# A convolution and two MLPs on one core: TensorE's program without a loop, and a reordered start

## The reference

```python
x (2, 4096, 192), weight (8, 7); moe_w_in (192, 2048), moe_w_out (2048, 192), and a second pair moe2_*
w = softmax(weight)                                   # one row of 7 taps for each group of 24 columns
x = sum over k of w[head, k] * x_padded[:, s + k]     # 6 rows of zeros ahead of each sequence
h = x @ w_in ;  g = maximum(0.01 * h, h) ;  x = g @ w_out
h = x @ w_in2 ; g = where(h >= 1, h, where(h <= -1, 0, (h + 1) ** 2 / 4)) ; out = g @ w_out2
```

## Time and profile before

| | us |
|---|---|
| median of 3 runs | 1184.76 (1181.87 to 1184.83) |
| the profiled execution | 1185.6 |
| its span, first to last instruction | 1183.9 |
| PE busy | 1161.6 (98%) |
| DVE busy | 896.6 (76%) |
| ACT busy | 798.2 (67%) |
| POOL busy | 50.6 (4%) |

### The profile page before, as it was taken

The page is one execution under the profiler, slowest core; times in us unless marked ns, Lnnn a source line. Parts: engine busy times, 40 slices in busy tenths (PEclk is TensorE's granted clock), DMA queues, the critical chain, the costliest instruction groups (busy, mean ns, idle before and its releaser), DMA issues.

```text
span 1183.9 us, 26785 instructions
## 1 busy us (share of the span) xinstructions
PE 1161.6 (98%) x9764; PEld 1142.1 (96%) x9764; DVE 896.6 (76%) x1509; ACT 798.2 (67%) x1473; POOL 50.6 (4%) x76
## 2 busy tenths in 40 slices
PE   9999999999999999999999999999999999999998
PEld 7879999999999999999999999999999999999997
DVE  6788777678777887768877678777777867878665
ACT  6768667485675857748577575765757657586685
POOL 5650000000000000000000000000000000000000
PEclk9999999999999999999999999999999999999999
DMA  5430100101001010010100101001010100100001
GB/s 136 109 61 2 18 11 1 30 2 25 4 2 30 2 28 2 2 29 2 28 2 10 22 2 28 1 12 19 1 28 1 25 7 1 28 1 16 1 1 28
DMA packets 114484, 22.43 MB, mean 19 GB/s; under 512 B 106128, under 2 KB 114320, under 8 KB 114320
## 3 DMA queue, kind: packets, MB, share of 16 engines
q1 hardware_dynamic: 114000, 20.07, 9.4%
q10 hardware_dynamic: 320, 0.26, 0.1%
HBM read 14.02 MB, written 6.29 MB: 17 GB/s over the span
## 4 chain that ended last, share of the span: by engine, by line
PE 93%; DVE 2%; ACT 2%; SPq 1%; issue 1%; POOL 0%; DMA 0%; POOLq 0%; ACTq 0%
PE hidden L385 7%; PE acc_main L477 5%; PE acc_main L479 5%; PE acc_main L475 5%; PE acc_edge L469 5%; PE acc_edge L467 5%; PE hidden L397 5%; PE hidden L401 5%; PE hidden L399 5%; PE hidden L404 5%; PE hidden L377 5%; PE hidden L381 5%; PE hidden L379 5%; PE acc_edge L441 5%; PE acc_edge L438 5%; PE acc_main L447 5%
## 5 line engine op out<-in xcount | busy, mean ns | idle before, releaser
L638 ACT CAST g_hi<-g 128x512 fp32r<-128x512 f32 x512 | 299.6, 618 | 311.5 <-PE acc_main L479 271.1
L848 DVE TENSOR_TENSOR g_lo<-g,g_hi 128x512 fp32r<-128x512 f32 x512 | 336.1, 690 | 143.9 <-ACT g_hi L638 138.9
L385 PE MATMUL hidden<-op_edge,w_edge 64*128 64x512 f32 x768 | 262.3, 395 | 0.0
L842 DVE SCALAR_TENSOR_TENSOR g<-hidden,pre 128x512 f32<-128x512 f32 x256 | 176.7, 690 | 105.7 <-ACT pre L626 102.8
L377 PE MATMUL hidden<-op_hi,w_main 64*128 64x512 f32 x512 | 202.3, 395 | 14.4 <-DVE g L837 13.8
L381 PE MATMUL hidden<-op_hi,w_main 64*128 64x512 f32 x512 | 202.0, 394 | 0.0
L441 PE MATMUL acc_edge<-g_lo,w_out 64*128 64x512 f32 x508 | 200.7, 395 | 1.0 <-DVE g_lo L848 0.8
L379 PE MATMUL hidden<-op_lo,w_main 64*128 64x512 f32 x512 | 201.7, 394 | 0.0
L397 PE MATMUL hidden<-op_hi,w_main 64*128 64x512 f32 x512 | 201.3, 393 | 0.0
L401 PE MATMUL hidden<-op_hi,w_main 64*128 64x512 f32 x512 | 201.3, 393 | 0.0
L399 PE MATMUL hidden<-op_lo,w_main 64*128 64x512 f32 x512 | 200.8, 392 | 0.0
(11 more groups left out here) (111 smaller groups left out, 2786.0 us busy)
## 6 DMA issues: line engine op xcount, KB each, us to landing
x_in<-in_x_dram SPq DMA_DIRECT2D x68, 64.0 KB, 2.2
out_dram<-y_main SPq DMA_DIRECT2D x64, 64.0 KB, 1.9
stage<-in_moe_w_out_dram SPq DMA_DIRECT2D x16, 192.0 KB, 3.5
x_in_edge<-in_x_dram SPq DMA_DIRECT2D x68, 32.0 KB, 1.9
out_dram<-y_edge SPq DMA_DIRECT2D x32, 64.0 KB, 1.8
stage<-in_moe_w_in_dram SPq DMA_DIRECT2D x15, 128.0 KB, 2.3
stage<-in_moe_w_in_dram SPq DMA_DIRECT2D x30, 64.0 KB, 3.0
stage<-in_moe_w_in_dram ACTq DMA_DIRECT2D x1, 128.0 KB, 3.2
```

Of the source, the lines that this page charges most:

```text
L385: done = nc.tensor.matmul(h[:], w_edge[l][top, i - 3, cols], op_edge[l][b][top, :], start=False, stop=False)
L638: nc.scalar.copy(g_hi[c % SLOTS][:], g[c % SLOTS][:]).then_inc(g_hi_ready, 1)
L848: nc.vector.tensor_tensor(g_lo[c % SLOTS][:], g[c % SLOTS][:], g_hi[c % SLOTS][:].bitcast(F32), ALU.subtract).then_inc(g_lo_ready, 1)
```

## The change

The diff has these parts.

- PE's program has no loop: the 7 passes are written out. The other engines keep theirs.
- The first warm-up has 12 matmuls instead of 8, the second 2 instead of 3, and the third (8, ahead of job 0) is gone.
- In `opening`, chunk 0 begins with its two edge passes and the edge pass of chunk 1, then come the passes with `op_hi`, and the ones with `op_lo` last. Each waits for its own operand. DVE instead of ACT makes two of the three edge operands of tile 0, in `edge_lo`, with a new semaphore `edge_tops_ready`.
- The two tap matmuls write to two banks, and ACT copies them one by one.
- Loads: the fourth quarter of the first `x_main` and `w_out` of piece 0 go from SP's queue to ACT's; the rest of piece 0 is issued behind the exponential; SP loads piece 2 ahead of the main part of tile 1.
- Jobs 0 and 1: the work for tile 1 and for the second MLP of tile 0 is laid at other chunks (`main_hi` at 5, `edge_hi` at 9, `edge_top` at 11, main taps at 0 to 3, edge taps at 2 to 8, `main_lo` at 7; in job 1 `take_edge` and what follows four chunks earlier, main taps from 9 instead of 7). Three main taps instead of two, and no edge taps, stand ahead of job 0. In the loop's jobs `turn`, `at` and `taps_at` give the chunks of before (`between_sum` at 10, and so on).

```diff
 AHEAD = 3
-WARM = 8
-WARM_ON = (3, 8)
+WARM = 12
+WARM_ON = 2
 EARLY = (0, 1)
...
         def _(sp):
-            def load_x_main(b, pos):
+            def load_x_main(b, pos, parts=P // Q):
                 group = b * (S // Q) + pos * GROUPS
-                for q in range(P // Q):
+                for q in range(parts):
                     sp.dma_start(x_in[b][Q * q:Q * (q + 1), :].rearrange("r (g c) -> r g c", c=Q),
...
-            load_x(EVEN, 0)
-            s, _, _, rows, _ = piece_parts(0)
-            sp.dma_start(rows, w_out_dram[0][:, 0:PC, :]).then_inc(stage_loaded[0], 16)
+            load_x_main(EVEN, 0, parts=P // Q - 1)
+            load_x_edge(EVEN, 0)
             load_weights(1)
+            load_weights(2)
             load_x_main(ODD, 0)
-            load_weights(2)
             load_x_edge(ODD, 0)
...
-            def top_first(job, c, i):
+            def top_first(job, c, i, first=0):
                 n, l, t, b = job["n"], job["layer"], job["t"], job["b"]
                 k = CHUNKS * n + c
                 cols = slice(c * P, (c + 1) * P)
                 h = hidden[c % SLOTS]
+                last = 1 if first else 4 - c % 2
+                done = None
+                if i == first and is_number(n, 0) and c % PC == 0:
+                    pe.wait_ge(weights_ready, c // PC + 1)
+                if first and c == 0:
+                    if i == first:
+                        pe.wait_ge(edge_tops_ready, 1)
+                    if i == 0:
+                        pe.wait_ge(main_rounded, 1)
+                    if i == 1:
+                        pe.wait_ge(first_main_ready, 1)
                 if i == 0:
-                    if is_number(n, 0):
-                        if c == 0:
-                            pe.wait_ge(first_main_ready, 1)
-                        if c % PC == 0:
-                            pe.wait_ge(weights_ready, c // PC + 1)
-                    elif c == 0:
+                    if c == 0 and not is_number(n, 0):
                         pe.wait_ge((op1_ready, op2_ready)[l], t + 1)
                     if reached(k, SLOTS):
                         pe.wait_ge(g_ready, k - SLOTS + 1)
-                    nc.tensor.matmul(h[:], w_main[l][top, 0, cols], op_hi[l][b][top, :], start=True, stop=False)
+                    nc.tensor.matmul(h[:], w_main[l][top, 0, cols], op_hi[l][b][top, :], start=first == 0, stop=False)
                 elif i == 1:
-                    nc.tensor.matmul(h[:], w_main[l][top, 0, cols], op_lo[l][b][top, :], start=False, stop=False)
+                    done = nc.tensor.matmul(h[:], w_main[l][top, 0, cols], op_lo[l][b][top, :], start=False, stop=False)
                 elif i == 2:
                     nc.tensor.matmul(h[:], w_main[l][top, 1, cols], op_hi[l][b][top, :], start=False, stop=False)
                 else:
-                    if is_number(n, 0) and c == 0 and i == 3:
-                        pe.wait_ge(op1_ready, 1)
                     done = nc.tensor.matmul(h[:], w_edge[l][top, i - 3, cols], op_edge[l][b][top, :],
-                                            start=False, stop=False)
-                    if i == 4 - c % 2:
-                        done.then_inc(hidden_top_made, 1)
+                                            start=i == first, stop=False)
+                if i == last:
+                    done.then_inc(hidden_top_made, 1)
...
                     last = c % 2 == 0
+                    if is_number(n, 0) and c == 0:
+                        pe.wait_ge(op1_ready, 1)
                     done = nc.tensor.matmul(h[:], w_edge[l][bottom, 0, cols], op_edge[l][b][bottom, :],
...
-                for i in range(5):
-                    top_first(job, 0, i)
+                for c, i in (0, 3), (0, 4), (1, 3), (0, 0), (0, 2), (1, 0), (0, 1):
+                    top_first(job, c, i, first=3)
                 for i in range(2):
-                    top_first(job, 1, i)
-                for i in range(2):
-                    top_first(job, 1, i + 2)
+                    top_first(job, 1, 2 - i, first=3)
                     bottom_first(job, 0, i)
...
             for a in (0, 1):
-                last = nc.tensor.matmul(acc_main[0][:, a * TAPS:(a + 1) * TAPS], head_of[:, a, :], taps_head[:],
-                                        start=True, stop=True)
-            last.then_inc(taps_spread, 1)
-
-            keep_warm(WARM_ON[0])
+                nc.tensor.matmul((acc_main, acc_edge)[a][0][:, 0:TAPS], head_of[:, a, :], taps_head[:],
+                                 start=True, stop=True).then_inc(taps_spread, 1)
+
+            keep_warm(WARM_ON)
             pe.wait_ge(x_turned, 1)
             for i in range(TAPS):
                 pe.wait_ge(diag_ready, i + 1)
                 last = nc.tensor.matmul(hidden[3][:], diag[i], x_main[0][:, i:i + T], start=i == 0, stop=i == TAPS - 1)
             last.then_inc(main_convolved, 1)
-            keep_warm(WARM_ON[1])
-            all_jobs(pe, run)
+            for job in first_jobs:
+                run(job)
+            for j in range(PASSES):
+                for job in loop_jobs(j):
+                    run(job)
+            for job in last_jobs:
+                run(job)
             for i in range(10):
...
                 act.wait_ge(edge_tapped, TAPS * (t + 1))
-                nc.scalar.copy(e[0:EDGE, 0:HALF], conv[0:EDGE, :]).then_inc(edge_hi_ready, 1)
+                if t > 0:
+                    nc.scalar.copy(e[0:EDGE, 0:HALF], conv[0:EDGE, :]).then_inc(edge_hi_ready, 1)
                 nc.scalar.copy(top[EDGE:P, HALF:T], conv[EDGE:P, :]).then_inc(edge_hi_ready, 1)
-                nc.scalar.copy(e[0:EDGE, HALF:T], conv[EDGE:P, :]).then_inc(edge_hi_ready, 1)
+                if t > 0:
+                    nc.scalar.copy(e[0:EDGE, HALF:T], conv[EDGE:P, :]).then_inc(edge_hi_ready, 1)
...
                         round_weights(AHEAD + PIECES - 1 + c // PC)
+                    if is_number(n, 0) and c == 1:
+                        move_half(job["load"])
+                    if is_number(n, 0) and c == 5:
+                        main_hi(job["finish"])
                     if is_number(n, 0) and c == 9:
-                        main_hi(job["finish"])
                         edge_hi(job["finish"])
+                    if is_number(n, 0) and c == 11:
                         edge_top(job["finish"])
-                    if job["prev"] and job["prev"][0] == LEAKY and c == 9:
+                    turn = 5 if is_number(n, 1) else 9
+                    if job["prev"] and job["prev"][0] == LEAKY and c == turn:
                         take_edge(n - 1, 1 - job["a"])
                         round_between(job["prev"], n - 1, 1 - job["a"])
-                    if job["prev"] and job["prev"][0] == LEAKY and c == 11:
+                    if job["prev"] and job["prev"][0] == LEAKY and c == turn + 2:
                         top_smooth(job["prev"])
...
                         move_halo(job["load"])
-                    if job["load"] and c == job["at"] + 2 and not is_number(n, 0):
+                    if job["load"] and c == 6 and not is_number(n, 0):
                         move_half(job["load"])
             act.dma_start(taps_raw[:], weight).then_inc(taps_loaded, 16)
-            s = piece_parts(0)[0]
-            act.dma_start(s[:, 0:PW], w_in_dram[0][0:P, 0:PW]).then_inc(stage_loaded[0], 16)
+            act.dma_start(x_in[EVEN][P - Q:, :].rearrange("r (g c) -> r g c", c=Q),
+                          x_rows[:, 0:GROUPS, P - Q:P]).then_inc(x_loaded[EVEN], 16)
             act.wait_ge(taps_step, 2)
             nc.scalar.activation(taps_exp[:], taps_sub[:], ACT.Exp).then_inc(taps_exp_ready, 1)
+            s, _, _, rows, _ = piece_parts(0)
+            act.dma_start(s[:, 0:PW], w_in_dram[0][0:P, 0:PW]).then_inc(stage_loaded[0], 16)
             for r in (0, EDGE):
                 act.dma_start(s[r:r + EDGE, PW:2 * PW], w_in_dram[0][P:D, 0:PW]).then_inc(stage_loaded[0], 16)
             act.wait_ge(taps_spread, 1)
-            nc.scalar.copy(taps[:], acc_main[0][:, 0:2 * TAPS].rearrange("p (a k) -> p a k", a=2)).then_inc(taps_ready, 1)
+            nc.scalar.copy(taps[:, 0, :], acc_main[0][:, 0:TAPS]).then_inc(taps_ready, 1)
             act.wait_ge(same_step, 3)
             act.wait_ge(taps_ready, 1)
             for i in range(TAPS):
                 nc.scalar.activation(diag[i], same, ACT.Copy, scale=taps[:, 0, i:i + 1]).then_inc(diag_ready, 1)
-                if i == 3:
+                if i == 0:
+                    act.wait_ge(taps_spread, 2)
+                    nc.scalar.copy(taps[:, 1, :], acc_edge[0][:, 0:TAPS]).then_inc(taps_ready, 1)
+                    act.dma_start(rows, w_out_dram[0][:, 0:PC, :]).then_inc(stage_loaded[0], 16)
+                if i == 2:
                     move_half((0, EVEN, 0))
             round_weights(0)
+            round_weights(1)
             edge_hi((0, EVEN, 0))
             main_hi((0, EVEN, 0))
             edge_top((0, EVEN, 0))
```

(52 more changed lines are left out.)

## The result

| | before | after |
|---|---|---|
| median, us | 1183.85 (4 runs) | 1162.58 (4 runs, 1162.14 to 1162.92) |
| the profiled execution | 1185.6 | 1162.36 |
| its span | 1183.9 | 1160.6 |
| PE busy | 1161.6 (98%) | 1151.9 (99%) |
| job 2 starts | 85.50 | 83.50 |

The ratio is 0.9816 (95% interval 0.9803 to 0.9829): 21.3 us less by the medians. The forecast was 1159.5, the range 1156 to 1167. Of the 23.3 us by which the span is shorter, 21.1 lie between the start of job 2 and the job behind the loop (993.17 instead of 1014.24 us), 2.0 in the start, 0.2 behind the loop.

The account below looks back on a forecast made before the run. TensorE (PE) was taken as the bound, busy 1161.6 of 1183.9 us. From 1185.6 us, 21.2 for the loop and 4.1 for the start gave 1160.3, less 0.8 for the median: 1159.5, range 1156 to 1167.

Parts of the forecast that it names:

- The loop: PE's 7 passes: PE waits for its own code after six jumps back; writing them out takes off 21.2 us.
- the surplus: Loop time above full rate, 21.2 us: six jumps at about 2.5 us and four slow-clock stretches at about 1.5 us.
- another 0.8 us: Taken off the sum of 1160.3 because the median of three lay 0.8 us below the profiled execution.
- The straight code is fetched in time: PE's written-out passes: code 7 times as long is fetched at the loop body's rate, at no cost.
- The rival in which it isn't: PE's straight code not fetched in time: 1328 us if each of about 80 blocks showed 2.1 us; chance 0.03.
- The cover of ACT's and DVE's jumps: Pass starts: DVE's first `g` stays 1.1 us ahead of PE's chunk 4; cost zero, without cover up to 8 us.
- The warm-up: Start: warm-up 8 to 12 lies on the path, costs 1.25 us; split tap banks return 0.25, convolution ends 1.0 later.
- larger start: Rival: convolution 1.0 to 1.3 us earlier, all waits of jobs 0 and 1 gone; start 6.5, time 1157; chance 0.12.
- DVE in front of the first `g`: Start of job 0: DVE's 3.0 us list after `op_lo` gives first `g` at 18.2 to 18.85; chunk 4 0.7 us earlier.
- The spreading: Jobs 0 and 1, chunk 4 to job 2: moving work to other chunks wins 3.4 of 3.8 us lost.
- My sum for ACT: Jobs 0 and 1: pre, cast and weights at 1.1 us each plus 1.3 us on top stay near 4.4 per pair.
- The start in all: Everything before job 2: 0.7 plus 3.4 gives 4.1 us won, between 2 and 6.5.

Follow-up runs that it names:

- the two pairs of kernels: Kernel before against itself with only PE's 7 passes written out (1163.91 us); changed kernel against itself with PE's loop put back (1181.37 us).
- the short loops that need no fetching: Changed kernel plus six 4-turn PE loops of 16 to 1400 matmuls behind its last product; three idles each with 1000 and 1400, none in the four shorter.

## Why the prediction was right or wrong, point by point

**The loop: right, in mechanism and size.** The sum gave 21.2 us for the passes, the two traces 21.1 (1014.24 to 993.17). The wait's name was VectorE, its cause PE's code: shown by the kernel before with only PE straight, and by the short loops that need no fetching. By the medians of the two pairs of kernels the loop is worth 18.8 and 20.9 us. One thing was overlooked: how many jumps are followed by a slow stretch changes from run to run (four in the profile of before, three with the loop put back). I had subtracted the surplus of an execution with four of them, at 1.5 us each, and then another 0.8 us because it lay that much above the median. But these stretches go with the jumps: the four runs before spread over 3.0 us, the four after over 0.8, and there the median lies 0.2 us above the profiled execution. That is 1.0 of the 3.1 us between the forecast and the measured median.

**The straight code is fetched in time: right** (4 packets, no gap). The rival in which it isn't fell by 4 packets in 65 us and no idle time behind job 2.

**The cover of ACT's and DVE's jumps: right.** 1.1 us was foretold, 1.4 is there, and taking the jumps away changes nothing (1163.06).

**The warm-up: its place was right, its worth wrong.** The tap matmul came at 5.84, where I had 6.1. The convolution ended at 13.3, 0.5 us later than before where I had 1.0: the second warm-up has two passes less (0.71 us instead of 0.94), which the sum left out. And I took four more matmuls as a cost only. They also make sure that the convolution runs at the quick rate; in the profile without them it ended 1.3 us later. The rival of a "larger start" did not come: without the longer warm-up the tap matmul was 1.0 us earlier and nothing was won.

**DVE in front of the first `g`: right step, size 0.45 us off, and partly by luck.** `op_lo` was ready at 15.35, not 15.15, its list took 3.3 us to the first `g` (3.0), which began at 18.62, not 18.2. Chunk 4 at 19.42, not 18.95. The 0.2 us at `op_lo` hide two errors against each other: the convolution ended 0.5 us earlier than I had it, and `op_lo` waited 0.7 us for DVE's edge operands, which my sum had at nothing though the change gives DVE two of them more. These ran beside POOL as well: L850 took 0.87 us here and 0.42 at 43.11, when POOL was idle.

**The spreading: this is the step that failed.** I had 3.4 of the 3.8 us gone. The chunk-4-to-job-2 stretch went from 65.83 to 64.08: 1.8 us. The old losses went as I had them, but for 0.8 us at the end of job 1, and new ones of 1.2 us came in job 0. Two terms were missing, and both are VectorE's time beside POOL. In job 0 I counted DVE's work per pair of chunks and from rows without POOL. A pair of `g_lo` takes 1.83 us there instead of 1.28, comes late behind the taps, and PE waits 0.42 us at 22.98; 0.9 us are lost by chunk 6 and 0.3 more by chunk 8. In job 1 I gave the taps no price at all; the only tap row I had, 0.66 us, has its sum in PSUM. There the sum is in SBUF beside POOL and takes 1.33 us, which makes the last rounding late and with it POOL's last piece, for which PE waits at 83.50. With the sum in PSUM that loss is gone. My sum for ACT was also added wrongly: 1.1 + 1.1 + 1.1 + 1.3 is 4.6 us and not near 4.4, but no loss showed for it at the casts. The start in all gave 2.0 us where I had 4.1, at the lower bound of my range for it, and that is 2.1 of the 3.1 us between the forecast and the measured median.

## What to carry to other kernels

An idle of about 2 us on the bound engine at the top of each loop pass can be its own code, whatever the profile names; look whether the named producer was long done and whether the same job without a jump idles, and count the slow stretch of the clock behind it. Writing the loop out is worth it only when the body is too long to stay at hand: a body of 600 matmuls turned round for nothing, one of 1000 didn't. When work is moved to another engine, add it to that engine's own list in front of the result that the others wait for. When work is spread between chunks, price each piece by a row with its own operands' places and neighbours, and follow the list between two results rather than the sum per pair.

## What the runs showed of the hardware

- A jump leaves PE idle for 1.9 to 2.3 us in a body of some 1216 matmuls, 1.8 and 2.0 in one twice as long, 1.5 to 1.9 with 1000 and 0.8 to 1.2 with 1400 matmuls without waits, and not at all with up to 600. That the longest body pays less than the one of 1000 I can't explain.
- After such an idle of 2 us the granted clock falls to the lower level (1.2 GHz) in some cases and not in others (4 of 6, 3 of 6, and 2 of 2), each time for about 1.5 us of lost time. The idle's length does not decide it: 1.88 us had a fall behind it and 2.10 us had none. Behind the six idles of 0.8 to 1.9 us in the loops of plain matmuls it never fell.
- VectorE's 128x512 tap takes 0.73 us alone and 1.33 us beside POOL when both inputs are in SBUF, 0.74 beside POOL when one is in PSUM.
- Two `g_lo` in a row (both inputs in SBUF) take 1.28 us alone and 1.83 beside POOL. In one execution POOL's L348 took 1.21 us and the pair 1.83, in another L348 took 1.81 and the pair 1.29.
